# One step of GpSimd work moved by two units in the attention part of an attention + mixture-of-experts + MLP kernel

## The chip, the cores and the metric

The kernel runs on one core of a Trainium2 chip, in one launch. The metric is the device time of that launch in microseconds. The core's engines have their own instruction queues and run side by side: TensorE (PE; its weight loads are shown apart as PEld), VectorE (DVE), ScalarE (ACT), GpSimd (POOL), and SyncE (SP), which only issues DMAs here. They wait for each other through semaphores. Each engine runs its queue strictly in the order written.

## The reference

Three stages in float32, one after the other:

```python
# 1. attention: q, k, v are [4, 8, 576, 64]; tau is a scalar (0.02)
scores = scale * np.matmul(q, k.transpose(0, 1, 3, 2))          # 32 heads of 576 x 576
thresh = np.max(scores, axis=-1, keepdims=True) - tau
scores = np.where(scores >= thresh, scores, -1000000000.0)
scores = scores - np.max(scores, axis=-1, keepdims=True)
attn = np.exp(scores)
attn = attn / (np.sum(attn, axis=-1, keepdims=True) + 1e-09)
x = np.matmul(attn, v)                                          # then laid out as 2304 tokens x 512
# 2. mixture of experts, 8 experts, one expert for each token
logits = x @ w_gate + modality_bias[modality_id]
e_idx = np.argmax(logits, axis=1); gate_w = softmax(logits) at e_idx
out[mask] = gate_w[mask, None] * (np.maximum(x[mask] @ w1[e], 0.0) @ w2[e])   # for each expert e
# 3. MLP, d_ff = 2048
h = out @ w_in
g = h * (1.0 / (1.0 + np.exp(-1.702 * h)))
return g @ w_out
```

The change lies in stage 1 alone.

## The kernel before

**Pairs and units.** The 32 heads are worked in 16 pairs (`PAIRS`), two pairs to a quad (`QUADS` = 8). The 2 x 576 query rows of a pair are cut into nine units of 128 rows: units 0 to 3 belong to the first head (side 0), unit 4 holds the last 64 rows of both, units 5 to 8 belong to the second head (side 1). In the code `n` counts all 144 units, `i` is the place within a quad (0 to 17), `j` the pair within the quad and `u` = `i % U` the unit within the pair. Quad 0 is written out, quads 1 to 3 (pairs 2 to 7) are a hardware loop, quads 4 to 7 are written out again. Pairs are numbered 0 to 15 here.

**What one unit takes.** PE multiplies a query tile by the keys into PSUM (`s_ps`, L1455; four matmuls, eight for unit 4). DVE reads that PSUM tile, scales and negates it into `scores` and takes the row minimum (L990, "the read-out" below). POOL adds tau to that minimum (`thresh`, L705, 128 x 1). ACT takes the exponential (L1282). DVE multiplies the result by the mask `scores <= thresh` and sums it (L792, "the mask"), two units behind its read-out. PE transposes the masked probabilities (L1412) five units behind, ACT copies them out of PSUM, and at units 1 and 5 of the next pair PE multiplies them by the values (L1469).

**Getting the next pair ready.** For exact arithmetic each q/k tile is split into a rounded part and the rest. POOL does this in `split(pair, side)`: a cast (L644) and a subtraction (L646), which write `qk_parts`; 640 elements a partition for side 0 (query tiles 0 to 4), 512 for side 1 (tiles 5 to 8). PE turns one tile of the next pair in each unit (L1426, weight loads and matmuls that read `qk_parts`), between the transposes of the probabilities and the scores of that unit. So tiles 0 to 4 of the next pair are needed at units 0 to 4, and tile 5, the first of side 1, at unit 5: there PE waits for `parts_ready`. The turned keys are then copied by POOL with their two halves exchanged, in `swap(pair, j, side)`: two copies (L654, L656) into `k_swap`, which the second and fourth score matmul of every unit read. PE waits for side 0 of it at unit 0 and for side 1 at unit 4.

**What waits for what.** PE's score of unit n waits until the read-out of unit n-2 has been done (`low_ready`). The read-out is followed on DVE by the mask of two units before. SP's loads of the next q/k tiles wait for `parts_ready`, since there is one raw buffer.

**What else lies in these pairs.** In pairs 8 to 11 DVE also does the routing arithmetic of the first half of the tokens, in short operations: in pairs 8, 9 and 10 they stand before the read-out of unit 2 (`early_part`: `bias_of_rows`, `half_logits`, `early_expert`), in pair 11 before the read-out of unit 3 (`early_split`). In pair 14 POOL starts the gather of the first expert tile: `gather`, two indirect DMAs (L687, L689), stands before the `thresh` of unit 2 and again before the `thresh` of unit 7; POOL waits for the loads of the second at unit 1 of pair 15, ahead of `swap`. In pair 14 and 15 DVE and ACT split the first expert's weights (L921, L1231).

POOL's step (L692 to L718) is the same loop over units; the split of side 1 stands in it at unit 0, the swap of side 1 at unit 1, the split of side 0 (for two pairs on) at unit 5 and the swap of side 0 (for the next pair) at unit 6.

Of the kernel before, what the change touches and what calls it, by code (L numbers as in the profile page):

```python
# [19 lines left out]
def attention_moe_mlp_kernel(nc, q, k, v, tau, modality_id, w_gate, modality_bias, w1, w2, w_in, w_out, out):  # L20
# [12 lines left out]
    PAIRS = NH // 2  # L33
# [41 lines left out]
    with ctx:  # L75
# [298 lines left out]
        def wait(eng, s, value):  # L374

            if not isinstance(value, int) or value > 0:
                eng.wait_ge(s, value)

        def on(value, low, high):

            return not isinstance(value, int) or low <= value < high
# [42 lines left out]
        def wait_apart(eng, s, value):  # L424


            if not isinstance(value, int):
                eng.wait_ge(s, value).then_inc(waited[eng.engine.name], 1)
            elif value > 0:
                eng.wait_ge(s, value)  # L430
# [202 lines left out]
        def _(pool):  # L633
            def split(pair, side):

                tiles = slice(0, TPB) if side == 0 else B_ROWS
                done = (pair * 2 + side - 1) * 2
                if side == 0:
                    wait(pool, qk_a_loaded, (pair + 1) * A_LOADS)
                    wait_apart(pool, turned, (pair - 1) * U + TPB)  # L640
                else:
                    wait(pool, qk_b_loaded, (pair + 1) * B_LOADS)
                    wait_apart(pool, turned, pair * U)
                pool.tensor_copy(qk_parts[:, tiles, :, 0], qk[:, tiles]).then_inc(parts_ready, 1)  # L644
                wait(pool, parts_ready, done + 1)
                pool.tensor_tensor(qk_parts[:, tiles, :, 1], qk[:, tiles], qk_parts[:, tiles, :, 0].bitcast(F32), ALU.subtract  # L646
                                   ).then_inc(parts_ready, 1)

            def swap(pair, j, side):

                wait_apart(pool, turned_copied, pair * U + (TPB if side == 0 else U))
                cols = slice(side * SEQ, (side + 1) * SEQ)
                done = pair * 4 + side * 2
                pool.tensor_copy(k_swap[j][0:DH, cols], qkT[j][DH:P, 1, cols]).then_inc(k_swapped, 1)  # L654
                wait_apart(pool, k_swapped, done + 1)
                pool.tensor_copy(k_swap[j][DH:P, cols], qkT[j][0:DH, 1, cols]).then_inc(k_swapped, 1)  # L656
                wait_apart(pool, k_swapped, done + 2)
# [27 lines left out]
            def gather(index, at, i, rows=N):  # L685

                pool.indirect_dma_start(tile_x[:, i], None, x_dram[0:rows], bass.IndirectOffsetOnAxis(index[:, at + i:at + i + 1], 0)  # L687
                                        ).then_inc(tile_x_loaded, 16)
                pool.indirect_dma_start(tile_gate[:, i:i + 1], None, gate_dram[0:rows],  # L689
                                        bass.IndirectOffsetOnAxis(index[:, at + i:at + i + 1], 0)).then_inc(tile_x_loaded, 16)  # L690

            def step(quad):  # L692
                for i in range(STEPS):
                    n = quad * STEPS + i
                    j, u = i // U, i % U
                    pair = quad * 2 + j
                    if isinstance(quad, int) and quad == QUADS - 1 and i in (2, 7):
                        pool.wait_ge(x_stored[0], PAIRS // 2 * 4 * 16)
                        pool.wait_ge(gate_stored, 4 * 16)
                        pool.wait_ge(early_list_ready, 1)  # L700
                        gather(early_list, 0, (2, 7).index(i), N // 2)
                    if on(n, 0, UNITS):
                        wait(pool, low_ready, n + 1)
                        wait(pool, probs_ready, n + 1 - STEPS)
                        pool.tensor_tensor(thresh[:, j, u:u + 1], row_low[:, j, u:u + 1], taus[:, 4:5], ALU.add  # L705
                                           ).then_inc(thresh_ready, 1)
                    if u == 0 and on(pair, 0, PAIRS - 1):
                        split(pair + 1, 1)
                    if isinstance(quad, int) and quad == QUADS - 1 and i in (6, 10):
                        pool.wait_ge(tile_x_loaded, (6, 10).index(i) * 32 + 32)  # L710
                    if u == 1 and on(pair, 0, PAIRS):
                        wait_apart(pool, thresh_ready, n + 1)
                        swap(pair, j, 1)
                    if u == 5 and on(pair, 0, PAIRS - 2):
                        split(pair + 2, 0)
                    if u == 6 and on(pair, 0, PAIRS - 1):
                        wait_apart(pool, thresh_ready, n + 1)
                        swap(pair + 1, 1 - j, 0)  # L718

            over_quads(pool, step, QUADS)  # L720

            for tile in range(1, EARLY):
# [998 lines left out]
```

## Time and profile before

| | us |
|---|---|
| time, median of 3 runs (1023.47 to 1024.69) | 1024.29 |
| the profiled execution's own time | 1023.47 |
| its span in the trace | 1021.9 |
| PE busy | 978.9 (96%) |
| DVE busy | 508.9 (50%) |
| ACT busy | 449.0 (44%) |
| POOL busy | 257.4 (25%) |

Around the span lie 1.57 us that the trace does not show. Attention runs from about 11 us to 351 us, the experts to about 611 us and the MLP to the end. A line of a timeline gives the start, the duration, the engine, the source line, the operation and its tiles; in brackets how long the engine was idle before it and what released it. The busy times of PE overlap, since matmuls are pipelined and their ends modelled, so a busy PE can still be waited for or be waiting for a fraction of a microsecond; the start of a weight load is the sharper mark.

### The profile page before, as it was taken

The page shows a single profiled execution, that of the slowest core. Times are in us where ns is not written, and L with a number is a line of the kernel's source. Part 1 is how long each engine was busy: PE and PEld are TensorE (multiplying, and loading weights), DVE is VectorE, ACT ScalarE, POOL GpSimd, SP SyncE. Part 2 cuts the span into 40 slices and gives each one's busy share as a digit, 9 for nine tenths or more (in the row PEclk, how much of TensorE's full clock was granted, in tenths as well). Part 3 has the DMA queues.
Part 4 walks back from the last instruction along what each step waited for, and adds up shares of the span by engine and source line. Part 5 has one row for each costly group of instructions (what it writes and reads, how often), then busy time and mean ns, then how long its engine had stood idle before and what let it go on. Part 6 is the DMA issues. An engine that isn't in the chain of part 4 may idle for free.

```text
span 1021.9 us, 18968 instructions
## 1 busy us (share of the span) xinstructions
PE 978.9 (96%) x6508; PEld 870.9 (85%) x6509; DVE 508.9 (50%) x1134; ACT 449.0 (44%) x1013; POOL 257.4 (25%) x358
## 2 busy tenths in 40 slices
PE   6999999999999996999999999999999999999994
PEld 5778878777787786999999999989999999999994
DVE  6888788899889673311114245522222222222221
ACT  4778777777788512311214254422222222222221
POOL 5664655456564204211112100010010100100101
PEclk8999999999999998999999999999999999999998
DMA  3232223222344116611110633210100101000000
GB/s 82 50 67 62 52 64 70 48 47 53 85 111 127 45 31 198 206 41 41 41 59 24 226 111 96 60 43 1 32 31 0 51 11 31 31 0 0 31 1 31
DMA packets 106936, 61.08 MB, mean 60 GB/s; under 512 B 87405, under 2 KB 95619, under 8 KB 106883
## 3 DMA queue, kind: packets, MB, share of 16 engines
q1 hardware_dynamic: 96195, 44.36, 16.1%
q0 software_dynamic: 4192, 10.51, 3.3%
q10 hardware_dynamic: 6496, 5.54, 1.7%
q8 instruction: 28, 0.46, 0.2%
q14 instruction: 25, 0.20, 0.1%
HBM read 45.68 MB, written 14.70 MB: 59 GB/s over the span
## 4 chain that ended last, share of the span: by engine, by line
PE 62%; DVE 2%; DMA 2%; issue 1%; POOL 1%; ACT 0%; POOLq 0%; ACTq 0%
PE s_ps L1679 19%; PE s_ps L1662 13%; PE s_ps L1520 10%; PE pt_ps L1662 7%; PE misc L1602 6%; PE o_ps L1602 5%; PE pt_ps L1512 1%; PE o_ps L1469 1%; DMA tile_gate<-gate_dram,early_list 1%; PE pt_ps L1412 1%; DMA tile_gate<-gate_dram,tile_index 1%; DMA tile_index<-order_dram 0%; POOL out_dram L746 0%; DVE row_hot L1054 0%; PE s_ps L1629 0%
## 5 line engine op out<-in xcount | busy, mean ns | idle before, releaser
L1174 DVE TENSOR_TENSOR g<-s_ps,sig 128x384 f32<-128x384 f32 x96 | 53.5, 557 | 279.2 <-ACT sig L1383 279.2
L1383 ACT ACTIVATE sig<-s_ps 128x384 f32<-128x384 f32 x96 | 47.2, 492 | 273.4 <-PE s_ps L1679 273.4
L990 DVE TENSOR_SCALAR_CACHE_REDUCE scores<-s_ps,taus 128x576 f32<-128x576 f32 x144 | 117.7, 817 | 46.5 <-PE s_ps L1455 26.2
L792 DVE SCALAR_TENSOR_TENSOR probs<-scores,thresh,probs 128x576 f32<-128x576 f32 x144 | 138.3, 961 | 0.0
L1412 PE MATMUL pt_ps<-ident,probs 128*128 128x128 f32 x720 | 127.1, 278 | 4.0 <-ACT pT L1197 1.4
L1679 PE MATMUL s_ps<-yT_high,w_in_high 128*128 (+1 forms) x384 | 129.5, 337 | 0.3 <-issue 0.2
L1679 PE MATMUL s_ps<-yT_high,w_in_low 128*128 (+1 forms) x384 | 129.5, 337 | 0.0
L1679 PE MATMUL s_ps<-yT_low,w_in_high 128*128 (+1 forms) x384 | 129.0, 336 | 0.0
L746 POOL DMA_INDIRECT out_dram<-out_sb,table x18 | 18.6, 1032 | 419.9 <-ACT out_sb L1358 416.3
L1282 ACT ACTIVATE probs<-scores,row_low 128x576 f32<-128x576 f32 x144 | 114.9, 798 | 17.6 <-DVE scores L990 16.2
L1412 PEld LDWEIGHTS pt_ps<-ident,probs 128*128 128x128 f32 x720 | 83.2, 141 | 29.2 <-issue 18.7
L1455 PE MATMUL s_ps<-qkT 128*128 128x288 f32 x320 | 102.5, 337 | 4.9 <-DVE scores L990 1.9
L705 POOL TENSOR_TENSOR thresh<-row_low,taus 128x1 f32<-128x1 f32 x144 | 74.0, 515 | 126.8 <-DVE scores L990 114.9
L1469 PE MATMUL o_ps<-pT,vv 128*64 128x320 f32 x640 | 93.2, 437 | 0.0
L1520 PE MATMUL s_ps<-xT_high,w_high 128*128 128x256 f32 x320 | 91.2, 285 | 1.1 <-issue 1.1
L1520 PE MATMUL s_ps<-xT_low,w_high 128*128 128x256 f32 x320 | 90.5, 283 | 0.0
L1520 PE MATMUL s_ps<-xT_high,w_low 128*128 128x256 f32 x320 | 90.5, 283 | 0.0
L1455 PE MATMUL s_ps<-k_swap,qkT 128*128 128x288 f32 x320 | 89.7, 296 | 0.0
L1197 ACT COPY pT<-pt_ps 128x512 f32<-128x512 f32 x144 | 84.9, 589 | 8.1 <-PE pt_ps L1412 4.6
L1679 PEld LDWEIGHTS s_ps<-yT_high,w_in_high 128*128 128x128 f32 x384 | 72.2, 188 | 5.1 <-issue 1.0
L1662 PE MATMUL s_ps<-w_out_high,g_low 128*128 128x512 f32 x192 | 76.2, 397 | 0.0
L1662 PE MATMUL s_ps<-w_out_low,g_high 128*128 128x512 f32 x192 | 75.8, 395 | 0.0
(258 smaller groups left out, 2186.1 us busy)
## 6 DMA issues: line engine op xcount, KB each, us to landing
w_raw<-in_moe_w_dram SPq DMA_DIRECT2D x24, 512.0 KB, 4.3
yT_dram<-tile_yT ACTq DMA_DIRECT2D x10, 512.0 KB, 3.1
x_dram<-xs SPq DMA_DIRECT2D x32, 128.0 KB, 2.2
w_in_raw<-in_moe_w_in_dram SPq DMA_DIRECT2D x4, 1024.0 KB, 5.4
w_out_raw<-in_moe_w_out_dram SPq DMA_DIRECT2D x16, 256.0 KB, 2.6
qk<-in_k_dram SPq DMA_DIRECT2D x30, 128.0 KB, 2.4
next_yT<-yT_dram SPq DMA_DIRECT2D x5, 768.0 KB, 4.5
qk<-in_q_dram SPq DMA_DIRECT2D x16, 128.0 KB, 2.1
```

Of the source, the lines that this page charges most:

```text
L705: pool.tensor_tensor(thresh[:, j, u:u + 1], row_low[:, j, u:u + 1], taus[:, 4:5], ALU.add).then_inc(thresh_ready, 1)
L792: dve.scalar_tensor_tensor(out=probs[:, i % PROB_SLOTS, 0:SEQ], in0=scores[:, i % SCORE_SLOTS], scalar=thresh[:, j, u:u + 1], in1=probs[:, ...
L990: dve.tensor_scalar(scores[:, i % SCORE_SLOTS].rearrange("p (c n) -> p c n", c=2), s_ps[i % 2][:, :, 0:HALF], taus[:, 3:4], None, ALU.mult ...
L1197: act.copy(pT[:, 0:TAIL, v * P:(v + 1) * P], pt_ps[:, 0:TAIL]).then_inc(keys_copied, 1)
L1282: act.activation(probs[:, k % PROB_SLOTS, 0:SEQ], scores[:, k % SCORE_SLOTS], ACT.Exp, bias=row_low[:, k // U, k % U:k % U + 1], scale=-1. ...
L1412: return pe.transpose(pt_ps[:, block], probs[:, k % PROB_SLOTS, block * P:(block + 1) * P], ident[:])
L1455: mm = pe.matmul(s_ps[i % 2][:, c, 0:HALF], qkT[j][:, 0, q_tile * P:(q_tile + 1) * P], keys[:, first:first + HALF], start=(at == 0), stop= ...
L1469: mm = pe.matmul(o_ps[lo:lo + DH, 0:UP], vv[j][:, side, block], pT[:, block, at:at + UP], start=(block == 0), stop=(block == TPB - 1))
L1520: mm = pe.matmul(hT_ps[f // 2][:, f % 2 * T:(f % 2 + 1) * T], w_part[:, a, f * P:(f + 1) * P], x_part[:, a], start=(a == 0 and part == 0), ...
L1602: mm = pe.matmul(yT_ps[d // 2][:, d % 2 * T:(d % 2 + 1) * T], w_part[:, f, d * P:(d + 1) * P], h_part[:, f], start=(at == 0 and part == 0) ...
L1662: mm = pe.matmul(mlp_y_ps[i], g_part[:, f % GT, at], w_part[:, f, :], start=(f == 0 and part == 0), stop=(f == FB2 - 1 and part == 2))
L1679: mm = pe.matmul(mlp_h_ps[f % 2], w_part[:, a, f * P:(f + 1) * P], y_part[:, bass.ds(c % 2 * DB + a, 1)].rearrange("p a b -> p (a b)"), st ...
```

## The change

In POOL's step the call `split(pair + 1, 1)` moves from unit 0, where it stood right behind the `thresh` of that unit, to unit 2, behind the `thresh` of that one and so behind `swap(pair, j, 1)` of unit 1. It holds for pairs 0 to 14. No instruction is added or taken away, and no other engine's order changes.

```diff
@@ -704,13 +704,13 @@
                         wait(pool, probs_ready, n + 1 - STEPS)
                         pool.tensor_tensor(thresh[:, j, u:u + 1], row_low[:, j, u:u + 1], taus[:, 4:5], ALU.add
                                            ).then_inc(thresh_ready, 1)
-                    if u == 0 and on(pair, 0, PAIRS - 1):
-                        split(pair + 1, 1)
                     if isinstance(quad, int) and quad == QUADS - 1 and i in (6, 10):
                         pool.wait_ge(tile_x_loaded, (6, 10).index(i) * 32 + 32)
                     if u == 1 and on(pair, 0, PAIRS):
                         wait_apart(pool, thresh_ready, n + 1)
                         swap(pair, j, 1)
+                    if u == 2 and on(pair, 0, PAIRS - 1):
+                        split(pair + 1, 1)
                     if u == 5 and on(pair, 0, PAIRS - 2):
                         split(pair + 2, 0)
                     if u == 6 and on(pair, 0, PAIRS - 1):
```

POOL's queue in pair 0, units 0 to 2, before (L705 is `thresh`, L644 and L646 the split, L654 and L656 the swap; in brackets the semaphores that a row waits for):

```order
L705 TENSOR_TENSOR thresh<-row_low,taus 128x1 [waits low_ready,tau_ready]
L644 CAST qk_parts<-qk 128x8x64 [waits turned,qk_b_loaded]
L646 TENSOR_TENSOR qk_parts<-qk,qk_parts 128x8x64 [waits parts_ready]
L705 TENSOR_TENSOR thresh<-row_low,taus 128x1 [waits low_ready]
L654 COPY k_swap_55<-qkT_53 64x576 [waits turned_copied,thresh_ready]
L656 COPY k_swap_55<-qkT_53 64x576 [waits k_swapped]
L705 TENSOR_TENSOR thresh<-row_low,taus 128x1 [waits low_ready,k_swapped]
```

The same stretch of POOL's queue now:

```order
L705 TENSOR_TENSOR thresh<-row_low,taus 128x1 [waits low_ready,tau_ready]
L705 TENSOR_TENSOR thresh<-row_low,taus 128x1 [waits low_ready]
L654 COPY k_swap_55<-qkT_53 64x576 [waits turned_copied,thresh_ready]
L656 COPY k_swap_55<-qkT_53 64x576 [waits k_swapped]
L705 TENSOR_TENSOR thresh<-row_low,taus 128x1 [waits low_ready,k_swapped]
L644 CAST qk_parts<-qk 128x8x64 [waits turned,qk_b_loaded]
L646 TENSOR_TENSOR qk_parts<-qk,qk_parts 128x8x64 [waits parts_ready]
```

The two rows of the split now stand behind three `thresh` rows and the swap; the swap has moved up by two rows. The other pairs read alike, with one exception.

POOL's queue in pair 14, from the `thresh` of unit 0, before (`tile_x` and `tile_gate` are the indirect DMAs of the gather):

```order
L644 CAST qk_parts<-qk 128x8x64 [waits turned,qk_b_loaded]
L646 TENSOR_TENSOR qk_parts<-qk,qk_parts 128x8x64 [waits parts_ready]
L705 TENSOR_TENSOR thresh<-row_low,taus 128x1 [waits probs_ready,low_ready]
L654 COPY k_swap_55<-qkT_53 64x576 [waits turned_copied,thresh_ready]
L656 COPY k_swap_55<-qkT_53 64x576 [waits k_swapped]
L687 DMA tile_x<-x_dram,early_list 128x512 [waits gate_stored,early_list_ready,x_stored0,k_swapped]
L689 DMA tile_gate<-gate_dram,early_list 128x1
L705 TENSOR_TENSOR thresh<-row_low,taus 128x1 [waits probs_ready,low_ready] x5
```

The same stretch now:

```order
L654 COPY k_swap_55<-qkT_53 64x576 [waits turned_copied,thresh_ready]
L656 COPY k_swap_55<-qkT_53 64x576 [waits k_swapped]
L687 DMA tile_x<-x_dram,early_list 128x512 [waits gate_stored,early_list_ready,x_stored0,k_swapped]
L689 DMA tile_gate<-gate_dram,early_list 128x1
L705 TENSOR_TENSOR thresh<-row_low,taus 128x1 [waits probs_ready,low_ready]
L644 CAST qk_parts<-qk 128x8x64 [waits turned,qk_b_loaded]
L646 TENSOR_TENSOR qk_parts<-qk,qk_parts 128x8x64 [waits parts_ready]
L705 TENSOR_TENSOR thresh<-row_low,taus 128x1 [waits probs_ready,low_ready] x4
```

Here the split, which stood ahead of both indirect DMAs, stands behind them.

## Rows read from the trace of the kernel before

The columns of a windows row are: the stretch, its length, busy us (instructions) of PE, PEld, DVE, ACT and POOL, the granted TensorE clock as a share of 2.4 GHz, the share of the DMA engines, GB/s.

**Rows 1.** windows, one pair each, from `thresh` of unit 0 to the next

```profile
71.78:91.65 19.87, 19.87 (x157) 15.90 (x153) 16.34 (x41) 15.80 (x41) 11.30 (x18) 1.00 0.27 61
214.89:237.77 22.88, 21.31 (x159) 16.32 (x157) 21.06 (x60) 16.25 (x41) 11.77 (x18) 1.00 0.24 53
```

**Rows 2.** timeline, pair 4, all engines (start us, duration us, ...)

```profile
90.66 0.82 DVE L990 TENSOR_SCALAR_CACHE_REDUCE scores<-s_ps,taus 128x576 f32<-128x576 f32 x1 [0.21 <-ACT probs L1282]
92.21 0.61 POOL L644 CAST qk_parts<-qk 128x512 fp32r<-128x512 f32 x1
92.89 1.27 POOL L646 TENSOR_TENSOR qk_parts<-qk,qk_parts 128x512 fp32r<-128x512 f32 x1
93.21 1.56 DVE L792 SCALAR_TENSOR_TENSOR probs<-scores,thresh,probs 128x576 f32<-128x576 f32 x1
95.10 0.29 PE L1455 MATMUL s_ps<-k_swap,qkT 128*128 128x288 f32 x1
95.54 0.82 DVE L990 TENSOR_SCALAR_CACHE_REDUCE scores<-s_ps,taus 128x576 f32<-128x576 f32 x1 [0.76 <-PE s_ps L1455]
99.27 0.25 PEld L1426 LDWEIGHTS pt_ps<-ident,qk_parts 128*128 128x128 f32 x2
```

**Rows 3.** timeline, start of attention

```profile
11.73 1.53 POOL L646 TENSOR_TENSOR qk_parts<-qk,qk_parts 128x640 fp32r<-128x640 f32 x1
13.32 0.69 PE L1426 MATMUL pt_ps<-ident,qk_parts 128*128 128x128 f32 x2 [1.69 <-POOL qk_parts L646]
```

**Rows 4.** timeline, pair 0, DVE and PE

```profile
17.54 0.82 DVE L990 TENSOR_SCALAR_CACHE_REDUCE scores<-s_ps,taus 128x576 f32<-128x576 f32 x1 [1.72 <-PE s_ps L1455]
20.01 0.82 DVE L792 SCALAR_TENSOR_TENSOR probs<-scores,thresh,probs 128x576 f32<-128x576 f32 x1
27.29 0.66 PE L1412 MATMUL pt_ps<-ident,probs 128*128 128x128 f32 x4 [0.84 <-DVE probs L792]
```

**Rows 5.** timeline, DVE and PE in pair 8 (first row) and pair 10

```profile
174.75 0.68 DVE L811 TENSOR_SCALAR mod_zero<-mod_one 128x18 f32<-128x18 f32 x1
219.93 0.82 DVE L990 TENSOR_SCALAR_CACHE_REDUCE scores<-s_ps,taus 128x576 f32<-128x576 f32 x1
220.90 0.37 PE L1455 MATMUL s_ps<-qkT 128*128 128x288 f32 x1 [0.90 <-DVE scores L990]
222.72 0.20 PEld L1426 LDWEIGHTS pt_ps<-ident,qk_parts 128*128 128x128 f32 x2
```

**Rows 6.** timeline, DVE and PE in pair 11

```profile
244.36 0.82 DVE L990 TENSOR_SCALAR_CACHE_REDUCE scores<-s_ps,taus 128x576 f32<-128x576 f32 x1
245.24 0.40 PE L1455 MATMUL s_ps<-qkT 128*128 128x288 f32 x1 [0.59 <-DVE scores L990]
```

**Rows 7.** timeline, pair 14: POOL, PE, DVE

```profile
305.32 1.34 POOL L687 DMA_INDIRECT tile_x<-x_dram,early_list  x1 [0.30 <-POOL k_swap L656]
306.89 0.25 PEld L1426 LDWEIGHTS pt_ps<-ident,qk_parts 128*128 128x128 f32 x2
306.96 1.40 POOL L689 DMA_INDIRECT tile_gate<-gate_dram,early_list  x1 [0.30 <-issue]
307.72 0.29 PE L1455 MATMUL s_ps<-k_swap,qkT 128*128 128x288 f32 x1
309.91 0.82 DVE L990 TENSOR_SCALAR_CACHE_REDUCE scores<-s_ps,taus 128x576 f32<-128x576 f32 x1 [0.23 <-DVE probs L792]
312.01 0.29 PE L1455 MATMUL s_ps<-k_swap,qkT 128*128 128x288 f32 x1
312.53 0.81 DVE L990 TENSOR_SCALAR_CACHE_REDUCE scores<-s_ps,taus 128x576 f32<-128x576 f32 x1
```

**Rows 8.** chain that ended last, second gather

```profile
317.40 5.86 DMA tile_gate<-gate_dram,early_list
```

**Rows 9.** windows of 1 us, columns as in rows 1: first and last of four

```profile
371.00:372.00 1.00, 1.00 (x6) 1.00 (x6) 0.83 (x6) 0.00 (x0) 0.00 (x0) 0.50 0.00 0
374.00:375.00 1.00, 1.00 (x9) 1.00 (x8) 0.85 (x5) 0.00 (x0) 0.00 (x0) 0.81 0.00 0
```

## The prediction

> **What bounds the kernel now.** I read the windows by pair first. In most pairs TensorE is busy from end to end: 19.87 us of a pair's 19.87, VectorE 16.34 [rows 1]. In pairs 8 to 11, where VectorE also does routing arithmetic, it is VectorE that sets the pace: pair 10 takes 22.88 us, with VectorE busy for 21.06 and TensorE for 21.31 [rows 1]. POOL is busy for a little over half a pair everywhere, so only when its results arrive can matter. Next I read the timeline of one steady pair, to see what the moved split touches on either side [rows 2], then the same places in the pairs that differ: 0, 8 to 11 and 14 [rows 4 to 7]. Last, the chain that ended last: it runs through the second gather of pair 14, 5.86 us on the DMA queue, back into attention [rows 8], and from there through TensorE and the routing arithmetic to the end. A delay inside attention therefore has nothing behind it to be swallowed by.
>
> **The change, part by part.** No instruction goes or comes; three things move. The split starts two units later, the swap of side 1 and `thresh` of unit 1 earlier, and in pair 14 the first gather comes ahead of the split.
>
> *The split's new arrival.* At unit 0 the cast began 1.55 us after the read-out began (92.21 - 90.66), and the subtraction ended at 94.16, so 3.50 us after it [rows 2]. Between lies `thresh`. The same three operations now follow the read-out of unit 2, so `qk_parts` is complete 3.50 us after that read-out begins. TensorE starts 0.06 us after a subtraction that it waits for (13.26 to 13.32) [rows 3]: together 3.55 us.
>
> *Steady pairs (1 to 7, 12, 13).* The read-out of unit 2 begins at 95.54 and TensorE's first weight load of tile 5 at 99.27, 3.73 us later [rows 2]. The parts come at 99.09: 0.18 us to spare. Nothing is saved either. The mask of 1.56 us at unit 1 is one that waited for the subtraction: it ended 0.61 us after it (94.77 against 94.16) and takes 0.82 otherwise [rows 2, 4]. Without the split it ends 0.74 earlier, but the read-out of unit 2 was idle for 0.76 us before it, waiting for TensorE [rows 2]. The blocking moves to the mask after the read-out of unit 3, where it costs some 0.3 us, and TensorE's long value product of unit 5 covers that. I take 0 for the nine pairs. Bounds: -0.1 each; and +0.2 each if a short VectorE operation (the reciprocal's `row_sum_eps`, which now falls on the split) slips in between cast and subtraction and eats the 0.18.
>
> *Pair 0.* VectorE sets the pace here and the split was done before it mattered. Now the read-out of unit 2 begins at 17.54, the subtraction ends at 21.04, and the mask that ran from 20.01 to 20.83 ends at 21.04 + 0.61 = 21.65 [rows 4]: +0.82 us on VectorE. TensorE waits for VectorE's masks 6 us later, 0.84 us idle [rows 4], so the delay goes through. I take +0.8; bounds 0 and 0.85 (all of it absorbed, all of it passed on).
>
> *Pairs 8, 9, 10.* The read-out of unit 2 is late because VectorE is, and TensorE waits for it, 0.90 us in pair 10 [rows 5]. The mask at unit 1 is no longer blocked, so the read-out comes 0.74 earlier, at 219.19. But the parts then come at 219.19 + 3.55 = 222.74, and TensorE loaded tile 5 at 222.72 before [rows 5]. What the wait for the read-out gives back, the wait for the parts takes: 0 for the three. Bounds: -0.3 and +0.2 each. What is late next is named by that: not `scores` but `qk_parts`.
>
> *Pair 11.* The seven short operations of `row_inv` and `early_split` stand between the read-outs of units 2 and 3, exactly where the split now lies. One such operation, on 18 elements a partition, took 0.68 us beside a POOL copy [rows 5]. TensorE waited 0.59 us for the read-out of unit 3, which began at 244.36 [rows 6], so what they lose goes on the path. They can lose nothing, or be held for the whole subtraction, 1.27 us [rows 2]. I take +0.7, the row of the blocked operation. The Trainium skill, SBUF — State Buffer, Who interferes with whom, says that copies, casts and `tensor_scalar` with SBUF on both sides can need the port pair which GpSimd uses and that the later one then waits for the whole instruction. By that rule, if all those operations meet its conditions, the term would be 1.27 and the sum 0.6 higher; the row of 0.68 fits it, but no row shows the 9-element ones under a subtraction.
>
> *Pair 14.* Before, the split was done when the gather began at 305.32; the gather held POOL until 308.36 [rows 7], and the next `thresh` began 0.07 later. Now the gather comes first. It begins earlier by about 0.75 (1.95 us of split are gone from in front of it, but VectorE's blocked mask, a weight split and the PE's scores hold the swap for part of that): 304.57. It takes its 3.11 us, to 307.68; `thresh` adds 0.15, cast and subtraction 1.95 (92.21 to 94.16, rows 2), the signal 0.06: parts at 309.85. TensorE loaded tile 5 at 306.89 [rows 7]. It waits 2.96 us. Behind the wait stand unit 5's scores, the value product and all later units, as TensorE works in order. The score of unit 6 had its last matmul at 312.01 and the read-out began 0.52 later; a read-out that waits for nothing else begins 0.44 later (95.10 to 95.54) [rows 2, 7]. So 0.08 is absorbed and VectorE, `thresh` of unit 6, the swap and the second gather behind it move by 2.9 us, and the 5.86 us of that gather's DMA with them [rows 8]. I take +2.9. Bounds: 1.7 if the gather starts by the full 1.95 earlier (1.20 more than I take); 3.7 if it does not start earlier at all.
>
> *Other queues.* SP's three loads of the next side-1 tiles wait for the split and start about 4 us later; they are needed a pair (20 us) on. The swap of side 1 is done about 0.8 us earlier; that is spare.
>
> *Sum.* 0 + 0.8 + 0 + 0.7 + 2.9 = +4.4 us. The profiled execution took 1023.47 (span 1021.9 and 1.57 around it), so its like is 1027.9. It was the fastest of three runs; on the median of 1024.29 the sum gives 1028.7, which I predict.
>
> **The rivals.**
>
> *Each steady pair waits too.* The 0.18 us are the whole margin of nine pairs. For: a short operation can take it. Against: rows 2 give a margin, and operations on POOL are regular to 0.1 us. At 0.2 us a pair: +1.8, 1030.5.
>
> *TensorE's clock falls in pair 14.* For four windows from 371 us the granted clock is 0.50, at the last 0.81, that is 1.2 GHz for 3.4 us [rows 9], after TensorE had waited for VectorE and then done a run of narrow matmuls. A stand of 3 us at 307 could do the same; 3.4 us at half speed cost 1.7: 1030.4. Against: TensorE is full before and after. The Trainium skill, TensorE: Matmul & The Clock Gate, Why this matters for your kernels, has a rule on this side: idle gaps long enough between bursts of matmuls send the array back to its half rate.
>
> *The wait in pair 14 is largely hidden: no change.* VectorE is behind there: it read unit 5 at 309.91 though the score's last matmul began at 307.72 [rows 7]. With the wait the read-out comes at 307.72 + 2.96 + 0.44 = 311.12, only 1.2 later. If that lag, not the later units, sets the pace, and pair 0's delay is absorbed where TensorE takes over, pair 14 gives 1.2 and the whole 1025.5. Against: unit 6 has next to no lag.
>
> *Faster.* If in pairs 8 to 10 the parts are not waited for, VectorE's 0.74 us is a gain in each, 2.2 us: 1022.1. It decides at one point: whether TensorE comes to tile 5 later than 3.55 us after the read-out of unit 2. In pair 10 it came 2.79 after it (222.72 - 219.93), so it would not; and pair 14 would have to cost nothing.
>
> **How the numbers follow.** The forecast 0.50, steady pairs 0.15, clock 0.13, hidden 0.15, faster 0.07. About 0.2% (2.05 us) is what a measurement of this kernel can tell from no change. Slower by more than that: the first three, 0.78; within: the fourth, 0.15; faster: 0.07. The forecast's own bounds (pair 14 from 1.7, pair 11 and pair 0 from 0, up to 3.7, 1.27 and 0.85) reach from 1026.0 to 1030.1; the range goes on to 1025.3 for the hidden case and to 1031.5 for the two dear ones.
>
> **What would show it.** In pair 14 TensorE's wait before the weight load of tile 5, released by `qk_parts` L646, of about 3 us, with the first gather ahead of it; if it is under 1 us, the largest step is wrong. In pair 0 a mask of about 1.6 us after the read-out of unit 3, and everything after it 0.8 later. In steady pairs no wait for `qk_parts` and a length of 19.9 us; in pair 10 a wait for `qk_parts` in place of the one for `scores`. In pair 11 stretched short operations. The granted clock near 307 to 315 us tells of the second rival. A time under 1026.3 would make the forecast wrong, one under 1022.2 its sign.

## The result, and the profile after

| | before | after |
|---|---|---|
| time, median, us | 1024.49 (4 runs, 1023.47 to 1024.83) | 1031.84 (4 runs, 1031.55 to 1032.59) |
| the profiled execution, us | 1023.47 | 1031.82 |
| its span, us | 1021.9 | 1030.2 |
| PE / DVE / ACT / POOL busy, us | 978.9 / 508.9 / 449.0 / 257.4 | 982.1 / 507.6 / 449.5 / 259.9 |

The change makes the kernel slower: the ratio after to before is 1.0075, 95% interval 1.0057 to 1.0092. The ratios and intervals here and below come from the single runs and need not be the quotient of the two medians. The sign and the place were as forecast. The size was +7.35 us where +4.4 was forecast, and 1031.84 lies just above the range (1031.5).

The windows of the two pairs of [rows 1], now:

```profile
72.73:92.73 20.00, 19.90 (x155) 16.00 (x153) 16.01 (x41) 15.86 (x41) 11.59 (x17) 1.00 0.26 58
216.19:238.95 22.76, 21.34 (x159) 16.34 (x157) 20.94 (x60) 16.32 (x41) 11.73 (x18) 1.00 0.25 54
```

The steady pair has grown by 0.13 us, pair 10 has shrunk by 0.12. Neither explains several microseconds; they are found by the place.

Pair 14 on all engines, timeline, the answer to [rows 7] (in brackets the idle time before a row and what released it):

```profile
306.38 1.34 POOL L687 DMA_INDIRECT tile_x<-x_dram,early_list  x1 [0.29 <-POOL k_swap L656]
308.01 1.41 POOL L689 DMA_INDIRECT tile_gate<-gate_dram,early_list  x1 [0.30 <-issue]
309.61 0.61 POOL L644 CAST qk_parts<-qk 128x512 fp32r<-128x512 f32 x1
309.93 0.91 DVE L792 SCALAR_TENSOR_TENSOR probs<-scores,thresh,probs 128x576 f32<-128x576 f32 x1
310.30 1.65 POOL L646 TENSOR_TENSOR qk_parts<-qk,qk_parts 128x512 fp32r<-128x512 f32 x1
312.01 0.29 PEld L1426 LDWEIGHTS pt_ps<-ident,qk_parts 128*128 128x128 f32 x2 [3.45 <-POOL qk_parts L646]
312.01 0.69 PE L1426 MATMUL pt_ps<-ident,qk_parts 128*128 128x128 f32 x2 [3.21 <-POOL qk_parts L646]
313.91 0.82 DVE L990 TENSOR_SCALAR_CACHE_REDUCE scores<-s_ps,taus 128x576 f32<-128x576 f32 x1 [3.07 <-PE s_ps L1455]
```

The gather's second DMA ends at 309.42, then come `thresh` and the split, and the parts arrive at 311.95. TensorE's weight load had nothing to do for 3.45 us, its matmul for 3.21. The matmul pair behind the wait takes 0.69 us; the same form takes 0.38 a unit earlier. The windows of after over this place say why (columns as in rows 1; the granted clock is the third figure from the end):

```profile
308.00:310.00 2.00, 0.80 (x7) 0.56 (x5) 1.78 (x6) 2.00 (x4) 1.92 (x3) 1.00 0.47 131
310.00:312.00 2.00, 0.00 (x0) 0.00 (x0) 0.84 (x3) 0.25 (x1) 1.92 (x3) 0.90 0.01 0
312.00:314.00 2.00, 1.99 (x9) 1.71 (x11) 0.09 (x1) 1.05 (x3) 0.25 (x2) 0.50 0.00 0
314.00:316.00 2.00, 2.00 (x12) 0.94 (x12) 2.00 (x5) 0.16 (x1) 0.70 (x1) 0.75 0.00 0
```

The clock starts to fall inside the stand (the time in which TensorE has nothing to do), and TensorE comes out of it at 0.50, that is 1.2 GHz, until into the fourth window. The chain of waits that ended last tells the same; it had run through the second gather [rows 8], and now, in order of time (start, us, what), these are among its pieces:

```profile
310.30 1.66 POOL qk_parts L646
312.01 0.69 PE pt_ps L1426 x2
313.87 3.42 PE o_ps L1469 x20
```

The value product of twenty matmuls takes 3.42 us here; in pair 4 of the same kernel it takes 2.91.

Pair 0, VectorE, the answer to [rows 4]:

```profile
17.52 0.82 DVE L990 TENSOR_SCALAR_CACHE_REDUCE scores<-s_ps,taus 128x576 f32<-128x576 f32 x1 [1.72 <-PE s_ps L1455]
19.98 1.65 DVE L792 SCALAR_TENSOR_TENSOR probs<-scores,thresh,probs 128x576 f32<-128x576 f32 x1
```

The mask takes 1.65 us instead of 0.82, as worked out, and every read-out of pair 0 from unit 4 on is 0.80 to 0.81 later than before.

Pair 4, the answer to [rows 2]:

```profile
96.47 0.82 DVE L990 TENSOR_SCALAR_CACHE_REDUCE scores<-s_ps,taus 128x576 f32<-128x576 f32 x1 [1.34 <-PE s_ps L1455]
98.70 1.29 POOL L646 TENSOR_TENSOR qk_parts<-qk,qk_parts 128x512 fp32r<-128x512 f32 x1
99.31 1.30 DVE L792 SCALAR_TENSOR_TENSOR probs<-scores,thresh,probs 128x576 f32<-128x576 f32 x1
100.20 0.25 PEld L1426 LDWEIGHTS pt_ps<-ident,qk_parts 128*128 128x128 f32 x2
100.85 0.82 DVE L990 TENSOR_SCALAR_CACHE_REDUCE scores<-s_ps,taus 128x576 f32<-128x576 f32 x1 [0.24 <-POOL thresh L705]
```

The parts are complete 3.52 us after the read-out of unit 2 begins (99.99 - 96.47), 0.21 before TensorE loads tile 5, and it waits for nothing. What I had priced too low is the mask behind the read-out of unit 3: it is held until 100.61, and the read-out of unit 4 comes 0.48 later against its neighbour than before.

Pair 10, the answer to [rows 5]:

```profile
220.44 0.82 DVE L990 TENSOR_SCALAR_CACHE_REDUCE scores<-s_ps,taus 128x576 f32<-128x576 f32 x1
222.67 1.27 POOL L646 TENSOR_TENSOR qk_parts<-qk,qk_parts 128x512 fp32r<-128x512 f32 x1
224.00 0.44 PE L1426 MATMUL pt_ps<-ident,qk_parts 128*128 128x128 f32 x2 [0.68 <-POOL qk_parts L646]
```

The wait for `scores` has become one for `qk_parts`, 3.56 us after the read-out of unit 2 (3.55 was forecast). The pair wins 0.1 us by the exchange.

Pair 11, the answer to [rows 6]:

```profile
244.17 1.29 POOL L646 TENSOR_TENSOR qk_parts<-qk,qk_parts 128x512 fp32r<-128x512 f32 x1
244.36 1.13 DVE L899 TENSOR_SCALAR place_slot_i<-place_i 128x9 int32<-128x9 int32 x1
245.96 0.82 DVE L990 TENSOR_SCALAR_CACHE_REDUCE scores<-s_ps,taus 128x576 f32<-128x576 f32 x1
246.84 0.40 PE L1455 MATMUL s_ps<-qkT 128*128 128x288 f32 x1 [0.78 <-DVE scores L990]
```

One short operation on nine elements a partition is held to the end of the subtraction, 1.13 us; the same line's neighbours take 0.17. Since the read-out of unit 2 had come 0.79 earlier, only 0.42 is left.

All waits of PEld between 10 and 350 us for the parts, summed (us in total, times, longest); before they were 1.9 us, once:

```profile
PEld pt_ps L1426 <- POOL qk_parts L646: 9.2, 7, 3.4
```

### The profile page after: what moved, and what is told of

Same layout as the page of the kernel before. It is cut to its first block, busy times and chain, and to the rows that moved or that the text cites. A ratio compares the mean times of both kernels' runs of the same rounds, so it can differ in the third digit from the quotient of the medians.

```text
span 1030.2 us, 18968 instructions
## 1 busy us (share of the span) xinstructions
PE 982.1 (95%) x6508; PEld 873.9 (85%) x6509; DVE 507.6 (49%) x1134; ACT 449.5 (44%) x1013; POOL 259.9 (25%) x358
## 4 chain that ended last, share of the span: by engine, by line
PE 79%; DVE 7%; issue 6%; POOL 3%; ACT 2%; DMA 1%; POOLq 0%; DVEq 0%; SPq 0%; ACTq 0%
PE s_ps L1679 19%; PE s_ps L1662 13%; PE s_ps L1520 9%; PE pt_ps L1662 6%; PE o_ps L1469 6%; PE misc L1602 6%; PE o_ps L1602 5%; PE pt_ps L1412 5%; PE s_ps L1455 5%; DVE probs L792 3%; PE pt_ps L1426 2%; DVE scores L990 1%; PE pt_ps L1512 1%; POOL qk_parts L646 1%; ACT probs L1282 1%
## 5 line engine op out<-in xcount | busy, mean ns | idle before, releaser
L990 DVE TENSOR_SCALAR_CACHE_REDUCE scores<-s_ps,taus 128x576 f32<-128x576 f32 x144 | 117.7, 818 | 54.1 <-PE s_ps L1455 34.0
L792 DVE SCALAR_TENSOR_TENSOR probs<-scores,thresh,probs 128x576 f32<-128x576 f32 x144 | 136.0, 946 | 0.0
L705 POOL TENSOR_TENSOR thresh<-row_low,taus 128x1 f32<-128x1 f32 x144 | 76.0, 529 | 131.4 <-DVE scores L990 119.9
```

What stands on the lines that cost most here:

```text
L792: dve.scalar_tensor_tensor(out=probs[:, i % PROB_SLOTS, 0:SEQ], in0=scores[:, i % SCORE_SLOTS], scalar=thresh[:, j, u:u + 1], in1=probs[:, ...
L990: dve.tensor_scalar(scores[:, i % SCORE_SLOTS].rearrange("p (c n) -> p c n", c=2), s_ps[i % 2][:, :, 0:HALF], taus[:, 3:4], None, ALU.mult ...
```

## The experiments

All kernels but three (fill_14, gate_later and behind_8_11) differ only in which pairs have the split of side 1 at unit 2 (`late`); nothing is left out of the computation in any of them. The median of before differs a little between the chips and hours, so each kernel is set against the one beside it. The table gives, in us, how much later than before the read-outs (L990) of the profiled executions began at the start of a pair; the last column is the span less that of before. A kernel may be up to 0.8 off at its very first row, which has nothing to do with the change, so differences between columns count.

| kernel | pair 1 | 8 | 11 | 12 | 13 | 14 | 15 | last unit | span |
|---|---|---|---|---|---|---|---|---|---|
| after | .80 | 1.48 | 1.18 | 1.60 | 1.92 | 1.85 | 6.26 | 6.19 | +8.3 |
| after_again | .50 | 1.25 | .96 | 1.40 | 1.71 | 1.60 | 7.31 | 7.24 | +7.9 |
| fill_14 | .98 | 1.69 | 1.43 | 1.85 | 2.17 | 2.05 | 5.10 | 5.03 | +6.5 |
| fill_14_again | .92 | 1.60 | 1.31 | 1.73 | 2.06 | 1.94 | 4.99 | 4.92 | +5.7 |
| only_14 | .24 | .19 | .19 | .19 | .19 | .19 | 3.23 | 3.40 | +5.8 |
| only_14_again | .11 | .10 | .09 | .08 | .08 | .07 | 4.46 | 4.38 | +6.3 |
| all_but_14 | 1.19 | 1.92 | 1.65 | 2.07 | 2.38 | 2.28 | 2.27 | 2.21 | +3.2 |
| gate_later | 1.14 | 1.84 | 1.52 | 1.94 | 2.24 | 2.13 | 3.62 | 3.55 | +3.8 |
| only_0 | .63 | .61 | .64 | .64 | .66 | .65 | .64 | .65 | +1.0 |
| steady | .29 | 1.03 | 1.04 | 1.02 | 1.34 | 1.21 | 1.19 | 1.13 | +3.4 |
| only_8_11 | .12 | .12 | -.16 | .25 | .26 | .26 | .26 | .27 | +1.5 |
| behind_8_11 | .15 | .12 | .70 | 1.42 | 1.89 | 1.88 | 1.88 | 1.89 | +2.6 |

**only_14: pair 14 alone.**

```diff
-                    if u == 0 and on(pair, 0, PAIRS - 1):
+                    late = isinstance(pair, int) and pair in (14,)
+                    if u == 0 and on(pair, 0, PAIRS - 1) and not late:
                         split(pair + 1, 1)
...
+                    if u == 2 and on(pair, 0, PAIRS - 1) and late:
+                        split(pair + 1, 1)
```

> The split of side 1 stands at unit 2 in pair 14 alone; all other pairs as before. Theory A: pair 14 carries most of the loss, by a wait of TensorE of 3 to 3.5 us behind the gather and 3.4 us of half clock behind that wait: the read-outs from unit 6 of pair 14 on come 4.2 to 4.6 us later than before, and the whole is 4.3 to 6.5 us slower (1028.8 to 1031.0), the spread being what the clock does after attention. Rival B: the small delays of the other pairs put VectorE into another phase and are needed for the loss: then the read-outs move by 3 us or less and the whole by at most 3.

Measured: 1030.69 us (4 runs) beside 1025.37 of before, ratio 1.0042 (1.0025 to 1.0059). Pair 14 adds 3.04 us (0.19 to 3.23). Here the clock did not fall, as the windows show:

```profile
308.00:310.00 2.00, 0.00 (x0) 0.00 (x0) 1.19 (x3) 0.80 (x2) 1.92 (x3) 1.00 0.01 0
310.00:312.00 2.00, 1.65 (x13) 1.23 (x15) 0.52 (x1) 1.06 (x3) 0.59 (x3) 1.00 0.00 0
```

So the step of pair 14 as I had worked it out, 2.9 us, is right when the clock stays. Theory A's step of 4.2 to 4.6 did not come in this execution; but the median is 5.3 above before, more than the 3 of rival B.

**all_but_14**: the change in every pair but 14, `late = not (isinstance(pair, int) and pair == 14)`.

> Unit 2 in all pairs except pair 14, which keeps the split at unit 0. Theory A: the read-outs at the start of pair 14 come 1.85 us later than before, as in the changed kernel, and stay so to the end of attention: 1.5 to 2.5 us slower than before (1026.0 to 1027.0). Rival B: 4 us or more remain.

Measured: 1027.13 us (10 runs), ratio 1.0016 (1.0002 to 1.0029), +1.8 us beside 1025.37. Fourteen pairs together cost about 2 us, and pair 14 adds nothing (2.28 to 2.27). The medians of the two parts, +5.3 and +1.8, come near the +7.35 of the whole.

**fill_14**: the whole change, and TensorE has 30 transposes of a constant to do ahead of its wait in pair 14, so that it does not stand.

```diff
@@ PE's transposes of the next pair's tiles
+                if isinstance(m, int) and m == (PAIRS - 2) * U + TPB + U:
+                    wait(pe, turned_copied, m)
+                    for _ in range(30):
+                        pe.transpose(pt_ps[:, 2 * (TPB - 1) - 1], ident[:], ident[:])
```

> The changed kernel with 30 more transposes of the unit matrix on TensorE in pair 14, unit 5, just ahead of its wait for the parts; they go to a PSUM block that nobody reads and last about 3.3 us, as long as the wait. Theory A (the clock fell because TensorE stood still): the granted clock stays at 1.00 behind it, the read-out of unit 6 comes 1.4 to 1.6 us earlier than in the changed kernel, and the whole is 1 to 2.5 us faster than that (1029.3 to 1030.8), although it does more work. Rival B (the clock's price is hidden behind VectorE, which is late anyway): the time stays at 1031.8 or rises.

Measured: 1029.28 us (10 runs), ratio 1.0031 (1.0022 to 1.0041). With more work it is faster than after. To have both side by side, it was run once more next to the unaltered change.

**after_again and fill_14_again.**

> The changed kernel once more, on the same chip as the three below. Its pair 14 either has the half clock behind the wait (read-out of unit 6 6.2 us later than before) or, as the run with unit 2 in pair 14 alone had it, the same wait without a fall of the clock (4.8 us later). If the fall comes in some executions and not in others, the median lies between the two; theory A then expects 6 to 8 us over before.

> As before: the changed kernel with 30 idle transposes ahead of the wait in pair 14, now side by side with the changed kernel. Theory A (a stand of 3.2 us can cost the clock, in some executions): 0.5 to 2 us faster than the changed kernel. Rival B (the clock at that place has no part in the median): within 0.3 us of it.

Measured, on one chip: after_again 1031.59 us (5 runs, 1030.56 to 1032.4), fill_14_again 1028.68 us (5 runs), before 1024.59 (18 runs); ratios to before 1.0062 (1.0048 to 1.0076) and 1.0034 (1.0021 to 1.0048). The filled stand is 2.9 us faster, more than the 0.5 to 2 that I expected, and the slowest of its five runs is faster than the fastest of after_again. after_again, windows:

```profile
310.00:312.00 2.00, 0.24 (x1) 0.24 (x2) 0.60 (x2) 0.01 (x1) 1.94 (x3) 0.64 0.01 0
312.00:314.00 2.00, 2.00 (x9) 1.57 (x10) 0.34 (x1) 1.21 (x3) 0.01 (x1) 0.50 0.00 0
314.00:316.00 2.00, 2.00 (x10) 0.95 (x8) 2.00 (x5) 0.00 (x0) 0.70 (x1) 0.50 0.00 0
316.00:318.00 2.00, 2.00 (x12) 0.78 (x8) 0.36 (x1) 0.00 (x0) 0.00 (x0) 0.66 0.00 0
```

fill_14_again, PE, PEld and POOL, timeline:

```profile
308.73 3.44 PE L1429 MATMUL pt_ps<-ident 128*128 128x128 f32 x30
310.40 1.67 POOL L646 TENSOR_TENSOR qk_parts<-qk,qk_parts 128x512 fp32r<-128x512 f32 x1
312.12 0.20 PEld L1436 LDWEIGHTS pt_ps<-ident,qk_parts 128*128 128x128 f32 x2 [0.19 <-POOL qk_parts L646]
```

fill_14_again, windows:

```profile
312.00:314.00 2.00, 2.00 (x17) 1.34 (x17) 0.77 (x3) 1.21 (x3) 0.36 (x3) 1.00 0.00 0
```

The parts come as late as in after, TensorE is busy until 0.19 us before them, and its clock stays at 1.00, here and in fill_14. Pair 14 then adds 3.05 us, as in only_14 (3.04); with the stand left open it adds 4.41 in after and 5.71 in after_again, where the low stretch lasts longer, 6.8 us instead of 3.4. The wait and the clock are two separate terms: 3.05 for the one, 1.4 to 2.7 in the traces for the other. That is close to half of the time that TensorE worked at the low clock after the stand, 3.0 us in after and 5.6 in after_again.

**only_14_again**: is it chance that the clock stayed in only_14?

> Pair 14 alone once more, as in only_14, whose profiled execution kept TensorE's granted clock at 1.00 behind a stand of 3.2 us. Theory: the clock's fall behind such a stand happens in some executions and not in others (or not at all in this kernel, if the place of the stand by a fraction of a us matters): pair 14 adds 3.0 us where it does not fall, and 4.4 or more where it does, and the median lies 5 to 7 us above before. Rival: the fall never comes in this kernel, because it needs the 1.8 us that the pairs before are late in the whole change; then the profiled execution shows 1.00 again, pair 14 adds 3.0, and the median is 3 to 4 us above before.

Measured: 1029.83 us (5 runs, 1028.7 to 1030.57), before 1025.13 (21 runs), ratio 1.0045 (1.0031 to 1.0059). The same kernel, windows:

```profile
308.00:310.00 2.00, 0.00 (x0) 0.00 (x0) 1.06 (x3) 0.70 (x2) 1.92 (x2) 0.95 0.01 0
310.00:312.00 2.00, 1.77 (x7) 1.52 (x7) 0.00 (x0) 0.83 (x3) 0.47 (x3) 0.50 0.00 0
```

This time it fell, after a stand of 3.22 us (3.24 in only_14), and pair 14 added 4.39. The median is 4.7 above before, a little under the 5 to 7 of the theory. Whether the clock falls behind this stand differs between executions of one and the same code; the late pairs ahead are not needed for it.

**gate_later**: the whole change, but in pair 14 only `tile_x` of the gather stands ahead of the split, `tile_gate` behind it.

```diff
-                        gather(early_list, 0, (2, 7).index(i), N // 2)
+                        if i == 2:
+                            pool.indirect_dma_start(tile_x[:, 0], None, x_dram[0:N // 2], ...)
+                        else:
+                            gather(early_list, 0, 1, N // 2)
...
                     if u == 2 and on(pair, 0, PAIRS - 1):
                         split(pair + 1, 1)
+                    if isinstance(quad, int) and quad == QUADS - 1 and i == 2:
+                        pool.indirect_dma_start(tile_gate[:, 0:1], None, gate_dram[0:N // 2], ...)
```

> The changed kernel, but in pair 14 only the first indirect DMA of the gather (tile_x) stays ahead of unit 2; the second (tile_gate) is issued behind the split. If the gather ahead of the split makes the wait, the parts come 1.64 us earlier (one DMA of 1.34 and the gap of 0.30), TensorE's wait shrinks from 3.45 to about 1.8 us, the clock doesn't fall, and the read-outs from unit 6 of pair 14 on come 3.2 us later than before or less, against 6.2; the whole is 2.5 to 4 us faster than the changed kernel. If the wait had another cause, the read-outs stay where they were.

Measured: 1027.61 us (8 runs), ratio 1.0031 (1.0020 to 1.0041), 4.0 under after_again beside it. PEld and POOL, timeline:

```profile
310.74 0.21 PEld L1441 LDWEIGHTS pt_ps<-ident,qk_parts 128*128 128x128 f32 x2 [1.86 <-POOL qk_parts L646]
310.84 1.33 POOL L726 DMA_INDIRECT tile_gate<-gate_dram,early_list  x1 [0.16 <-issue]
```

With one of the two indirect DMAs taken out from in front of the split the stand is 1.86 us instead of 3.45, pair 14 adds 1.49 instead of 3.05, and the clock stays at 1.00. The read-outs from unit 6 on come 3.6 later than before, for the 3.2 or less that I expected, as the pairs ahead are 2.1 late here. It is the gather ahead of the split that makes the wait.

**only_0**: pair 0 alone.

> Unit 2 in pair 0 alone. Both: the mask after the read-out of unit 3 lasts about 1.65 us, and every read-out from unit 4 of pair 0 to the end of attention comes 0.8 us later. The whole is 0.8 us slower (1025.3) if the low stretch of the clock in the routing part stays as long as before, and up to 2 us more if a delay alone can lengthen it.

Measured: 1026.78 us (10 runs), ratio 1.0005 (0.9995 to 1.0015), which can't be told from no change. In the trace the step is plain: the read-outs of units 1 to 3 lie 0.17 to 0.22 ahead of before, that of unit 4 lies 0.62 behind it, a step of 0.84, and it stays until attention ends.

**steady**: pairs 1 to 7, 12 and 13 alone.

> The split of side 1 stands at unit 2 in pairs 1 to 7, 12 and 13 alone. Theory now: each of these pairs loses about 0.1 us, because the subtraction at unit 2 blocks the mask behind the read-out of unit 3 and the read-out of unit 4 comes late, and pair 12 about 0.3: read-outs +0.67 at the start of pair 8 and about +1.0 at the start of pair 14, and the time +1.0 us. Rival (the prediction's own 0): these pairs lose nothing and the growth seen with the whole change was carried over from pair 0; then +0.2 or less at the start of pair 8 and within 0.3 us of the kernel before. In both, TensorE waits nowhere over 0.3 us for qk_parts.

Measured: 1025.58 us (11 runs) beside 1025.13, ratio 1.0005 (0.9996 to 1.0014). In the trace the seven pairs cost 0.74 us (0.29 to 1.03) and pair 12 costs 0.32, of which pair 13 gives 0.13 back: the theory's sizes, though the median alone could not tell +1.0 from 0.5 or 0. The rival that this growth was carried over from pair 0 falls, since pair 0 is unchanged here. Where it comes from, VectorE in pair 3 of steady:

```profile
85.12 0.82 DVE L996 TENSOR_SCALAR_CACHE_REDUCE scores<-s_ps,taus 128x576 f32<-128x576 f32 x1 [1.05 <-PE s_ps L1461]
85.86 1.17 DVE L798 SCALAR_TENSOR_TENSOR probs<-scores,thresh,probs 128x576 f32<-128x576 f32 x1
87.27 0.82 DVE L996 TENSOR_SCALAR_CACHE_REDUCE scores<-s_ps,taus 128x576 f32<-128x576 f32 x1 [0.23 <-POOL thresh L705]
```

Since the read-outs of units 4 and 5 are late, POOL's split of side 0, which was not moved, is late by as much (its subtraction begins at 84.85, before at 84.24), while TensorE reaches unit 6 nearly in time. The mask at unit 6 is therefore held longer, 1.17 us instead of 0.94, and the read-out of unit 7 is 0.23 later against its neighbour. About half of that is left at the end of the pair. I have this from the rows alone; no run takes the second blocking away by itself.

**only_8_11**: pairs 8 to 11 alone.

> The split of side 1 stands at unit 2 in pairs 8 to 11 alone. Theory: pairs 8, 9 and 10 win 0.1 us each (the read-out of unit 2 comes 0.78 us earlier, the wait for the parts gives back 0.68), pair 11 loses 0.4: read-outs at the start of pair 11 -0.3, at the start of pair 12 +0.1, the time within 0.3 us of before. Rival: the gain of those pairs in the whole change was catching up on the delay that pair 0 and the steady pairs had brought; then 0 or more at the start of pair 11 and +0.4 to +0.7 at the start of pair 12.

Measured: 1024.65 us (11 runs) beside 1025.13, ratio 0.9995 (0.9986 to 1.0004): no change. The trace has -0.28 for pairs 8 to 10 (0.12 to -0.16) and +0.41 for pair 11, with no delay ahead of them to catch up on. No version with a gain that can be measured came out of this; the best part of the change is worth 0.3 us.

**behind_8_11**: in pairs 8 to 11 of the kernel before, the split goes to unit 1, right behind the swap, so that neither the mask of unit 1 nor the parts should be late.

```diff
+                    behind = isinstance(pair, int) and pair in (8, 9, 10, 11)
-                    if u == 0 and on(pair, 0, PAIRS - 1):
+                    if u == 0 and on(pair, 0, PAIRS - 1) and not behind:
                         split(pair + 1, 1)
...
+                    if u == 1 and on(pair, 0, PAIRS - 1) and behind:
+                        split(pair + 1, 1)
```

> Before, but in pairs 8 to 11 the split stands at unit 1, right behind the swap. The mask at unit 1 is no longer blocked, so the read-out of unit 2 (pairs 8, 9, 10) comes 0.78 us earlier, and the parts are ready about 1 us ahead of TensorE's need, as the routing arithmetic holds the read-out of unit 2. Theory: TensorE's waits for that read-out (0.24, 0.63 and 0.90 to 1.11 us in the three pairs, at most 0.78 each) go: read-outs 1.3 to 1.8 us earlier at the end of pair 11, and the whole 1 to 2 us faster than before. Rival: the swap's 1.5 us and the split then block the short operations and the next mask instead, and 0.3 us or less are left.

Measured: 1025.87 us (11 runs) beside 1024.59, ratio 1.0008 (0.9999 to 1.0017). The theory fell: the median shows no gain, and the trace a loss, 0.60 us in pair 8 and 0.72 in pair 11. Pair 9, DVE, POOL and PEld:

```profile
198.20 1.28 POOL L646 TENSOR_TENSOR qk_parts<-qk,qk_parts 128x512 fp32r<-128x512 f32 x1
198.57 1.52 DVE L798 SCALAR_TENSOR_TENSOR probs<-scores,thresh,probs 128x576 f32<-128x576 f32 x1
200.42 0.82 DVE L996 TENSOR_SCALAR_CACHE_REDUCE scores<-s_ps,taus 128x576 f32<-128x576 f32 x1
201.30 0.19 PEld L1461 LDWEIGHTS s_ps<-qkT 128*128 128x128 f32 x1 [0.38 <-DVE scores L996]
```

The read-out of unit 2 does come earlier, but the subtraction now lies under the mask behind it, that mask takes 1.52 us, and TensorE waits for the read-out of unit 3. Wherever the subtraction goes, some mask is held by it. How much that costs depends, as I read these rows, on whether VectorE has idle time behind that mask.

## Why the prediction was right and where it was wrong

*The split's new arrival* was right: 3.52 us after the read-out of unit 2 in pair 4 and 3.56 in pair 10, for 3.55.

*Pair 0*, +0.8: right, +0.81 in after and a step of 0.84 in only_0.

*Steady pairs* (1 to 7, 12, 13), 0: too low. They cost 0.1 each in pairs 1 to 7, and pairs 12 and 13 together 0.2 to 0.25, in all 0.9 us (steady: 0.29 to 1.21). The margin of 0.18 us that the text watched held. The cost came from the step beside it: that the longer mask after unit 3 would be covered by the value product of unit 5. It was not covered on POOL, which is fed by VectorE; this last link is read from rows, as said at steady.

*Pairs 8, 9, 10*, 0: -0.1 each, inside the bounds, and the exchange of one wait for the other was as told. *Pair 11*, +0.7: +0.42. The operation held was held for 1.13 us, nearer the bound of 1.27 than the 0.68 that I took, and the earlier read-out of unit 2, which I had left out, gave 0.79 back. The Trainium skill, SBUF — State Buffer, Who interferes with whom, has the port pair as a lock that goes to the one who starts first and holds the other to the end; the 1.13 us fit that, and so do the mask of pair 14 at 309.93, which began first and took 0.91, and the subtraction behind it, which took 1.65 instead of 1.29 (0.36 more, for 0.54 us under the mask).

*Pair 14*, +2.9: as the cost of the wait it was right, 3.05 with the clock held (fill_14, only_14), and gate_later shows that the gather in front makes it. The start of the gather was forecast 0.75 us earlier, and came so: 306.38 less the 1.85 of the pairs ahead is 304.53, for 304.57.

The measured terms of after add up: 0.80 + 0.93 - 0.30 + 0.42 + 3.05 + 1.36 (clock) = 6.26, the delay of the first read-out of pair 15. Without the clock they are 4.90, 0.5 above the forecast's 4.4; the misses of the steady pairs and of pairs 8 to 11 partly cancel, which is luck.

*The step that failed* is the one that priced pair 14's stand at its length alone and put the fall of TensorE's clock aside as a rival with a chance of 0.13, "against: TensorE is full before and after". The clock fell to 0.50 behind the stand in after, after_again and only_14_again, and not in only_14. Filling the stand, with the parts arriving as late as in after, makes the kernel 2.9 us faster in runs side by side, and that is the size of what was missing: fill_14 and fill_14_again lie 3.9 and 4.1 above the before beside them, for a forecast of 4.4. That the medians agree so closely is luck in part, since the traces of the two are 4.9 to 5.0 late at the end of attention. The rival's own price, 1.7, lies within the 1.4 to 2.7 of the traces of attention and under the 2.9 of the medians.

The range failed with it. The clock's price should have been added to the forecast's upper bounds, not set beside them: forecast and clock together, even at 1.7, gave 1030.4, with the upper bounds of the other terms 1031.8. *The hidden case and the faster case* did not come: unit 6's lag was as small as told, and in pair 10 the parts were waited for. Of the signs forecast for the profile, the stand in pair 14, the mask of pair 0, the wait for `qk_parts` in pair 10 and the stretched short operation in pair 11 are there.

What lies behind attention was no term of the sum, and its cause stays open. In after the last read-out is 6.19 us late and the span 8.3; in only_14 it is 3.40 and 5.8, with the clock whole in attention. The rows show where most of the rest arises. In after, the last 66 matmuls of the routing, `s_ps` L1629 and `misc` L1602, take 3.10 and 7.99 us for 2.42 and 7.10 before, and `order_rows`, which waits for them and starts the DMAs of the next expert tile, is 7.77 late. VectorE (first row before, second after), and the chain of after:

```profile
378.93 0.28 DVE L1109 CAST order_rows<-s_ps 18x128 uint32<-18x128 f32 x1 [0.52 <-PE s_ps L1635]
386.70 0.28 DVE L1109 CAST order_rows<-s_ps 18x128 uint32<-18x128 f32 x1 [2.08 <-PE s_ps L1635]
375.48 3.10 PE s_ps L1629 x18
378.57 7.99 PE misc L1602 x48
```

Over this stretch of matmuls the granted clock was 0.82 before and in after_again, 0.69 in after, only_14_again and steady, and 1.00 in only_14. Where it was 0.69, `order_rows` lost 1.5 to 1.6 us more; steady has no stand in pair 14 and has this loss all the same, so the stand is not what it needs. In only_14 the stretch was faster than before, and the growth lies in the DMAs between `order_rows` and the next tile, among them `tile_index` and `tile_gate`, 10.6 us together for 8.9. One profiled execution of each cannot tell whether a later end of attention changes these or whether they differ by chance. Of the 2.9 us between the medians of after_again and fill_14_again, the profiled pair has 2.3 at the last read-out; where the rest arises is not shown.

## What to carry to other kernels

A wait of some microseconds on an engine that was full can cost more than its length: here 3.05 us of waiting brought 1.4 to 2.7 more through TensorE's clock in three traces and nothing in a fourth, and the two have to be added, with their uncertainties, and not weighed as alternatives. When a step is moved down a queue, look first for the one place where something long (here two indirect DMAs, 3.0 us) lies between the old place and the new; one pair of fifteen made over two thirds of the loss in attention. And moving a POOL operation that blocks VectorE did not remove the blocking in any of these kernels: it must come to lie where VectorE has slack behind it, and the queues that VectorE feeds must be followed for a whole round.

## What the runs showed of the hardware that I had not expected

After a stand of 3.2 to 3.45 us at full load on both sides, the granted TensorE clock was 0.50 for about 3.4 us (after, only_14_again) or 6.8 us (after_again), and in one execution of four it did not fall at all (only_14, 3.24 us). The Trainium skill, TensorE: Matmul & The Clock Gate, Why this matters for your kernels, tells to leave no long gaps between bursts of matmuls; three traces agree, the fourth shows that such a gap need not bring the fall.

It can also come after less. In behind_8_11 TensorE waited in pair 11 for 0.31 and then 1.19 us, and the windows read:

```profile
244.00:246.00 2.00, 1.14 (x9) 0.66 (x6) 1.81 (x6) 0.00 (x0) 0.99 (x2) 1.00 0.02 4
246.00:248.00 2.00, 1.36 (x8) 0.94 (x10) 1.77 (x5) 1.38 (x4) 0.70 (x1) 0.89 0.57 129
248.00:250.00 2.00, 2.00 (x12) 0.82 (x10) 1.77 (x6) 1.09 (x3) 0.19 (x1) 0.50 0.02 2
```

The twenty matmuls of the value product took 4.60 us there, for 2.91 at full clock. The read-outs of that pair did not suffer, 1.40 late before it and 1.42 after it; but from unit 2 of pair 12 on they are 1.89 late, where only_8_11 has no such step (0.25 and 0.26). Whether that 0.47 is the clock's is not shown.

A mask held by a subtraction on POOL ends at a fixed distance behind it. In before, 23 masks began under a subtraction and were held; they took 0.88 to 2.05 us instead of 0.82, and each ended 0.60 to 0.63 us after its subtraction.

Thirty 128 x 128 transposes filled 3.44 us, 0.115 each, and kept the clock at 1.00.
